# Token product by seven block products instead of eight, with the sums on VectorE

## The reference, cut to what matters

```
x  = attention(q, k, v)                    # 2 x 768 x 512; a band of 96 keys and 8 global keys
t  = x @ w_theta;  zr, zi = x*cos(t), x*sin(t)
y  = w_tok_r @ zr + w_tok_i @ zi           # over the 768 tokens, for each of 2 batches
u  = x + y
v  = u + relu(u @ w_ch)
h  = relu(v @ w_in);  g = h * sigmoid(conv3(h))
out = g @ w_out                            # 2 x 768 x 512
```

## Time and profile before

| | |
|---|---|
| median of 3 runs | 404.9 us (404.44 to 405.19) |
| the profiled execution's own time | 405.32 us |
| its span in the trace | 403.6 us |
| TensorE matmul busy | 396.9 us (98%), 2268 instructions |
| VectorE busy | 214.4 us (53%) |
| ScalarE busy | 215.1 us (53%) |
| GpSimd busy | 130.0 us (32%) |
| DMA moved | 32.17 MB, mean 80 GB/s |

### The profile page before, as it was taken

The page is one execution under the profiler, slowest core; times in us unless marked ns, Lnnn a source line. Parts: engine busy times, 40 slices in busy tenths (PEclk is TensorE's granted clock), DMA queues, the critical chain, the costliest instruction groups (busy, mean ns, idle before and its releaser), DMA issues.

```text
span 403.6 us, 6205 instructions
## 1 busy us (share of the span) xinstructions
PE 396.9 (98%) x2268; PEld 348.2 (86%) x2268; DVE 214.4 (53%) x577; ACT 215.1 (53%) x414; POOL 130.0 (32%) x106
## 2 busy tenths in 40 slices
PE   7999999999999999999999999999999999999996
PEld 2888888898788888888888988999999999999985
DVE  5977777765888643448254421487434435344320
ACT  2777777764787544482333120588555544553531
POOL 2095000001567233265442210248562322222220
PEclk9999999999999999999999999999999999999999
DMA  7964442620000233235420002002100200100022
GB/s 229 417 256 161 162 161 80 144 97 2 0 1 5 101 98 138 78 123 190 132 78 1 2 0 78 28 2 73 31 2 0 80 0 1 52 29 2 0 78 78
DMA packets 12271, 32.17 MB, mean 80 GB/s; under 512 B 4176, under 2 KB 4432, under 8 KB 12240
## 3 DMA queue, kind: packets, MB, share of 16 engines
q1 hardware_dynamic: 12240, 31.77, 22.6%
HBM read 28.62 MB, written 3.15 MB: 79 GB/s over the span
## 4 chain that ended last, share of the span: by engine, by line
PE 96%; ACT 1%; DVE 1%; issue 1%; ACTq 0%
PE bank L453 32%; PE bank L594 24%; PE bank L652 16%; PE bank L500 9%; PE bank L485 6%; PE bank L472 5%; PE bank L565 1%; PE bank L608 1%; PE bank L511 1%; ACT pr L711 1%; DVE trig L1134 0%; ACT trig L779 0%; DVE th_r L1036 0%; DVE bank L1033 0%; DVE xT L1025 0%
## 5 line engine op out<-in xcount | busy, mean ns | idle before, releaser
L594 PE MATMUL bank<-z,wT 128*128 128x512 f32 x432 | 99.3, 390 | 0.0
L594 PEld LDWEIGHTS bank<-z,wT 128*128 128x128 f32 x432 | 80.8, 188 | 16.6
L453 PE MATMUL bank<-vT,win 128*128 128x386 f32 x384 | 73.3, 340 | 0.0
L453 PEld LDWEIGHTS bank<-vT,win 128*128 128x128 f32 x384 | 68.4, 188 | 1.8
L652 PE MATMUL bank<-wout,g 128*128 128x512 f32 x288 | 69.6, 390 | 0.0
L652 PEld LDWEIGHTS bank<-wout,g 128*128 128x128 f32 x288 | 53.9, 188 | 9.7
L1211 DVE SCALAR_TENSOR_TENSOR bank<-h_sb,convw,bank 128x384 f32<-128x384 f32 x32 | 19.9, 622 | 66.7 <-ACT bank L868 66.7
L862 ACT ACTIVATE h_sb<-bank 128x386 f32<-128x386 f32 x32 | 15.8, 493 | 74.0 <-PE bank L453 73.0
L415 POOL TENSOR_TENSOR g<-gf,g 128x384 fp32r<-128x384 f32 x32 | 32.5, 1017 | 68.0 <-ACT g L882 68.0
L500 PE MATMUL bank<-v_sb,pT 128*128 128x65 f32 x352 | 44.6, 268 | 0.0
L500 PEld LDWEIGHTS bank<-v_sb,pT 128*128 128x128 f32 x352 | 43.1, 192 | 0.0
(11 more groups left out here) (77 smaller groups left out, 496.1 us busy)
## 6 DMA issues: line engine op xcount, KB each, us to landing
wrows<-w_tok_laid SPq DMA_DIRECT2D x12, 768.0 KB, 4.4
v_sb<-v_laid SPq DMA_DIRECT2D x8, 780.0 KB, 5.0
qk_sb<-qk_laid SPq DMA_DIRECT2D x7, 792.0 KB, 6.5
out<-ob SPq DMA_DIRECT2D x12, 256.0 KB, 2.2
winraw<-w_in_in SPq DMA_DIRECT2D x4, 512.0 KB, 3.8
woutraw<-w_out_in SPq DMA_DIRECT2D x8, 256.0 KB, 2.7
wthraw<-w_theta_in SPq DMA_DIRECT2D x1, 1024.0 KB, 12.9
wchraw<-w_ch_in SPq DMA_DIRECT2D x1, 1024.0 KB, 5.2
```

Of the source, the lines that this page charges most:

```text
L453: last = pe.matmul(dst, w[a], m[b], start=(i == 0 and j == 0), stop=(i == n - 1 and j == 2))
L594: last = pe.matmul(Y_BANK[s % 2][:], wT[s % 2][:, hi, ri * NT + blk, :], z[b][:, blk, lo, ri, :], start=(blk == 0 and ri == 0 and j == 0), ...
```

## The change

The token product of both batches is written as a product of 2 x 2 blocks: on the left, rows are the two halves of the output tokens (0 and 1, 384 each) and columns the real and imaginary weights; on the right, rows are zr and zi and columns the two batches. Strassen's seven block products take the place of eight. A step `mix_tokens(s)` now has s = 3k + i with k from 0 to 6 (the product) and i from 0 to 2 (the tile in the half); its contraction is 6 blocks long: 18 matmuls of 128 x 512.

- **Left operands.** GpSimd's `prepare(i)` makes, for each i, the seven left operands (five sums or differences and two plain parts) from four raw rows of 768, during the attention: 9 two-input operations and 4 copies of 128 x 768. Six operands stay in SBUF (`a_ops`); five per i are staged, written to a DRAM tensor `a_kept` (`store_a`), and come back in the token stage (`load_a`); the last nine of them come as one part and are split by `high_a` (ScalarE) and `low_a` (VectorE). In exchange SP's `load_w_tok`, `high_rows`, `low_rows` and GpSimd's `split_rows` are gone. `load_v` has three buffers instead of two.
- **Right operands.** `weigh` writes into four raw arrays; `own_difference`, `other_difference`, `sum_six`, `sum_one`, `sum_seven` on VectorE (15 operations of 128 x 1024, SBUF and SBUF) make the sums; `high_b` (ScalarE) and `low_b` (VectorE) split them in 18 pieces of 128 x 1024. The first batch's `high_z` and `low_z` now take 512 columns; the second batch's are gone.
- **Results.** `add_y` adds or subtracts a bank to two tiles of x for k = 0 to 4 and to one for k = 5 and 6.
- **Mixed channels.** v stays in PSUM: `add_mix` is one operation, `high_v` and `low_v` read the bank, `low_v` moves from GpSimd to VectorE; `mix_channels` waits for `low_v`. `high_u` writes a second, unrounded copy (`u_raw`).
- **Orders.** New hand-written orders on TensorE, ScalarE and VectorE. w_in and w_out are loaded later (w_in after the last `low_b`, w_out after the last `add_mix`).

```diff
+        ADDS = (((1, ALU.add), (3, ALU.subtract)), ((1, ALU.add), (0, ALU.add)), ((2, ALU.add), (0, ALU.subtract)),
+                ((2, ALU.add), (3, ALU.add)), ((0, ALU.add), (3, ALU.add)), ((0, ALU.add),), ((3, ALU.add),))
+        B_RAW = (zi[0], zi[1], zd, zr[0], zi[0], zr[1])
...
+            def first_tokens():
+                pe.wait_ge(x_done, NU)
+                pe.wait_ge(staged, NA)
+                for blk in range(NT):
+                    pe.wait_ge(z_lo, blk + 1)
+                    for i in range(NI):
+                        for j, (hi, lo) in enumerate(((0, 0), (0, 1), (1, 0))):
+                            last = pe.matmul(y_bank(i)[:], a_ops[:, i, hi, blk, :], b_ops[:, b_side(0), blk, lo, :], ...)
...
+                for blk in range(NT):
+                    if k >= 1 and i == 0 and blk % 2 == 0:
+                        pe.wait_ge(b_lo, NI * (k - 1) + blk // 2 + 1)
+                    for j, (hi, lo) in enumerate(((0, 0), (0, 1), (1, 0))):
+                        last = pe.matmul(y_bank(s)[:], a_ops[:, slot, hi, blk, :], b_ops[:, side, blk, lo, :], ...)
...
-                if n >= 2:
-                    pe.wait_ge(v_ready, n - 1)
+                if n >= 2:
+                    pe.wait_ge(v_lo, n - 1)
```

GpSimd and its stores:

```diff
+                step(summed(resident(i), w_r1, w_i1, ALU.add))
+                whole(resident(NI + i), w_i1)
+                summed(kept(0), w_r0, w_i0, ALU.add).then_inc(staged, 1)
+                whole(kept(1), w_r0).then_inc(staged, 1)
+                for part, a, b, op in ((2, w_r0, w_i1, ALU.add), (3, w_i0, w_i1, ALU.subtract), (4, w_r1, w_r0, ALU.subtract)):
+                    pool.tensor_tensor(kept(part)[0].bitcast(F32), a, b, op).then_inc(staged, 1)
...
+                prepare(0)
+                prepare(1)
                 split_w_theta()
-                for s in range(2):
-                    split_rows(s)
+                prepare(2)
...
+                for p, count in zip(range(3, NP), (0, 5, 1, 4, 5)):
+                    load_qk(p)
                     load_v(p)
+                    for m in range(kept, kept + count):
+                        store_a(m)
+                        if m == 4:
+                            load_w_raw(2)
```

VectorE's work and its order (the start of it), and ScalarE's wait ahead of the angles:

```diff
+            def low_b(k, two):
+                dve.wait_ge(b_hi, NI * (k - 1) + two + 1)
+                dve.tensor_tensor(b_ops[:, b_side(k), blks, 1, :], B_RAW[k - 1][:, blks, :],
+                                  b_ops[:, b_side(k), blks, 0, :].bitcast(F32), ALU.subtract).then_inc(b_lo, 1)
...
+                dve.scalar_tensor_tensor(out=r, in0=r, scalar=0.0, in1=u_raw[:, j, :], op0=ALU.max, op1=ALU.add)\
+                   .then_inc(v_ready, 1)
...
+            weigh(6)
+            own_difference(0)
+            own_difference(1)
+            own_difference(2)
+            low_b(1, 0)
+            low_b(1, 1)
+            weigh(7)
+            low_b(1, 2)
...
+                if t == 0:
+                    act.wait_ge(staged, NA)
+                    for m in range(4):
+                        act.wait_ge(stored_a[m], 16 * ((NA + 3 - m) // 4))
```

More of the change, by code:

```diff
@@ L28, with build @@
 PI_BELOW = 3.1415925
-def build(nc, q, k, v, qk_laid, v_laid, counts, w_theta, w_tok, w_ch, w_in, conv_w, w_out, out):
+def build(nc, q, k, v, qk_laid, v_laid, counts, w_theta, w_tok, w_ch, w_in, conv_w, w_out, a_kept, out):
     B, H, S, D = q.shape
@@ L634, in hidden @@
                 cols = slice(0, HC) if half == 0 else slice(S - HC, S)
-                product(H_BANK[n % 2][:, 0:HC], [([win[:, part, blk, f * P:(f + 1) * P] for part in range(2)],
+                product(H_BANK[n % 2][:, 0:HC], [([win[blk][:, part, f * P:(f + 1) * P] for part in range(2)],
                                                   [vT[b][:, part, blk, cols] for part in range(2)])
@@ L1153, in _ @@
                     weigh(TRIG_AT[t])
-            for m in range(NT):
-                if m >= 1:
-                    add_y(m - 1)
-                    low_rows(m + 1)
-                weigh(NT + m)
             def low_u(c, blks=range(CB)):
@@ new lines, in _ @@
+            weigh(6)
[6 more added lines that the diff above has]
+            low_b(1, 2)
+            weigh(8)
+            weigh(9)
+            add_y(0)
+            weigh(10)
+            weigh(11)
+            low_b(2, 0)
+            add_y(1)
+            other_difference(0)
+            low_b(2, 1)
+            low_b(2, 2)
+            add_y(2)
+            add_y(3)
+            add_y(4)
@@ L1187, in _ @@
+            add_y(9)
+            sum_one(0)
+            sum_one(1)
+            low_v(1)
+            sum_one(2)
+            low_b(4, 0)
+            add_y(10)
+            add_y(11)
+            low_a(6)
+            low_b(4, 1)
+            low_b(4, 2)
             add_mix(2)
             add_mix(3)
+            low_a(7)
+            low_v(2)
+            low_v(3)
             low_u(1)
-            add_y(8)
-            low_rows(10)
+            add_y(12)
+            sum_seven(0)
+            low_a(8)
@@ L1192, in _ @@
+            sum_seven(1)
+            sum_seven(2)
             add_mix(4)
             add_mix(5)
-            add_y(9)
-            low_rows(11)
+            low_v(4)
+            add_y(13)
+            low_b(5, 0)
+            low_v(5)
+            low_a(9)
+            low_a(10)
+            low_b(5, 1)
+            low_b(5, 2)
+            add_y(14)
+            low_a(11)
+            low_a(12)
+            low_b(6, 0)
+            add_y(15)
+            add_y(16)
+            low_b(6, 1)
@@ L1196, in _ @@
+            low_b(6, 2)
             add_mix(6)
             add_mix(7)
+            low_v(6)
+            low_a(13)
+            add_y(17)
+            low_a(14)
             low_u(2)
-            add_y(10)
-            add_y(11)
+            low_v(7)
+            add_mix(8)
+            add_y(18)
+            low_v(8)
+            add_mix(9)
+            low_v(9)
+            add_mix(10)
+            add_mix(11)
+            low_v(10)
+            low_v(11)
+            add_y(19)
+            add_y(20)
```

581 lines of the change are left out of this document (357 added, 224 removed).

## The result

The changed kernel takes 395.09 us (median of 4 runs, 394.86 to 395.29), the kernel before in the same session 404.67 (404.44 to 405.19): a ratio of 0.976, 95% interval 0.974 to 0.978. The forecast was 394.9. In a later session (5 runs, and 11 of the kernel before) it was 394.74 to 405.07, 0.975 (0.974 to 0.976). With 0.976 in its place the differences to the changed kernel would be 0.4 us smaller, so they are good to about that.

The account below looks back on a forecast made before the run. TensorE was taken as the bound, time being matmuls times the distance of their starts. Saving 12.2 us, less 2.2 of waits, attention at zero, gave -10.0: from 404.9 to 394.9 us, range 392.5 to 399.8.

Parts of the forecast that it names:

- Bound, matmuls removed: Token product: TensorE sets the time; 378 matmuls instead of 432, 54 fewer at 0.2267 us, save 12.2 us.
- VectorE's list: Token stage: VectorE's operations take 93.6 us against TensorE's 114.5, so the order decides; no TensorE wait up to 244.
- The place named as the tightest: Token stage, transpose_u(1): needed at 188.3, add_y(11) there at 187.7, 0.6 us to spare.
- spare of 0.6 to 2 us: Token stage up to 244: how far ahead of TensorE's need the walk had its inputs ready.
- The overlap that I chose: VectorE's list in the token stage: 0.06 us taken off for each of 84 wide operations, 98.6 down to 93.6 us.
- The four late waits: TensorE behind 244: mix_channels(3,0) waits 0.35, mix_channels(3,2) 0.56, hidden(7) 0.40, hidden(8) 0.85; together 2.2 us.
- the last pair: Waits at hidden(7) and (8), 0.40 and 0.85 us, from the relu, taps, sigmoid, gate loop with a w_out split.
- The attention at zero: Attention: GpSimd's three prepares, 19.8 us each from 19.4, end with w_theta at 85 to 87, hidden; cost zero.
- The 0.6 us wait in the angle stage: TensorE's longest wait behind the start-up; the only possible gain there, as high_z and low_z get shorter.
- VectorE as the pace, early or throughout: Rivals: VectorE paces the token stage, part given back (0.24); or it becomes the bound, slower than before (0.04).
- the rival's two parts: Rival (0.24): two-SBUF operations 1.16 times as long lose 3.1 us, hand-overs of 0.15 us lose 2.5; both: 400.5.
- The fall of the clock: Rival (0.02): many small TensorE waits bring one 13 us stretch to 1.2 GHz, costing 13 us: 408.

Follow-up runs that it names:

- before_378: The kernel before with 378 of its 432 token matmuls, one low-by-high product left out for 9 of 12 tiles: 393.29 us, ratio 0.970.
- eighth_product: The changed kernel with the first block product (54 matmuls) computed twice into the same banks: 407.62 us, ratio 1.005 to the kernel before.
- woven_early: The changed kernel with channel mixes between hiddens, early first w_out pieces and splits, and the last two high_u ahead of the first sigmoid: 392.51 us, ratio 0.969.
- woven: The changed kernel with one mix_channels(3,j) between each two of hidden(3) to hidden(8), w_out loaded as late as in the changed kernel: 396.79 us, ratio 0.979.
- prepare_load: The changed kernel with three more two-input operations of 128 x 768 on GpSimd in prepare(2): 400.68 us, ratio 0.988 to the kernel before.
- vector_load: The changed kernel with 12 more VectorE subtractions of 128 x 768, two ahead of each low_b of products 3 and 4: 403.27 us, ratio 0.994.

## Why the prediction was right

- **Bound, matmuls removed.** Right: 54 x 0.2267 = 12.2; before_378 gives 12.1 and eighth_product 12.3.
- **VectorE's list.** Right in sum, and in place but for one: 93.6 foretold, 92.3 us busy between 134 and 244; no wait on TensorE from the first token matmul to `hidden(0)`, which starts at 244.0. The place named as the tightest has the spare foretold: `add_y(11)` ends at 187.1, `transpose_u(1)` starts at 187.75. But there is a tighter one, which the list leaves out and my "spare of 0.6 to 2 us" doesn't cover, and that it went without a wait is partly luck: `mix_channels(2,2)` starts at about 235.7 and needs the `low_v` that ends at 235.5, `mix_channels(2,3)` at about 237.8 one that ends at 237.6. These four mixes follow one another, so v's way through ScalarE and VectorE takes all but 0.2 us of the time; it is the chain that costs 0.4 at `mix_channels(3,2)`. The overlap that I chose, 0.06 a piece, is 0.085 for the `low_b`.
- **The four late waits.** Right: 2.2 foretold, 2.1 by the timeline, 2.2 by woven_early. Of the cause given for the last pair, the late start behind the load holds: with load and splits moved ahead both waits go. That the loop also carries a split doesn't matter: without one its relus are just as far apart, 2.97 us against 2.95.
- **The attention at zero.** Right in the result, and nearly wrong in the reason. A prepare takes 20.6 us (42.50 - 21.88) and not 19.8, from the hand-overs between its operations, and GpSimd starts at 21.9, for it waits for its raw rows behind the other loads, where I had let it start at 19.4. The last operation ends at 90.3 where the sum had 85 to 87, and the sign of being right, done before 90, failed. The last store was to be down at 90; it is down at about 93, and the stage needed it at 93.5. The spare that I gave as 4 us was under a half, and that the cost still came out as nothing is luck: two terms missing from the sum, 2.5 us of hand-overs and a start 2.5 us later, had just used it up. The 0.6 us wait in the angle stage, which I had allowed to go, stayed.
- **Sum and rivals.** 10.0 foretold, 9.6 and 10.3 measured in two sessions. VectorE as the pace, early or throughout, did not come about: its wide operations kept to 1.22 us but for the hits by GpSimd. The upper end of the range, 399.8, also lay below the 400.5 that the rival's two parts give together, though it was to take the rival in. The fall of the clock did not come about in the changed kernel, whose waits are all under a us; it is real, though, as woven and prepare_load show, and I had given it as something that many small waits bring, where here it followed single ones of 2.9 and 4.8 us.

## What to carry to other kernels

Where one engine is at its limit, removed instructions are worth their distance in full, and the work put in their place is free only where the other engine has time left, which the mean over the stage doesn't tell: VectorE had 4% left in one half and 28% in the other, and 11.4 us more of work, two thirds of it in the first, cost 8. (No run loaded the second half, so its room isn't shown.) Walk the ordered lists against each other with durations from rows; here it gave the four waits to 0.2 us. Walk every wait in the source, also those between rows of one kind: the tightest was one that had been left out. An order change should be walked together with the loads that hang on it (woven against woven_early). Where work is taken as hidden under other work, start it from when its data has landed, and add the hand-overs between its own operations.

## What the runs showed that I had not expected

- A wait of TensorE can cost more than itself. After 2.9 us without matmuls (woven) the next 9 took 3.8 us instead of 2.2; after 4.8 us (prepare_load) the next 12 took 4.3 instead of 3.0, with the granted clock at 0.61 and 0.57 of full in those stretches, so at the 1.2 GHz level for part of them. In the changed kernel and vector_load, with waits of 0.4 to 1.4 us, it stayed at full. The Trainium skill, TensorE: Matmul & The Clock Gate, section "HAM oscillation", has the fall to half rate behind waits between bursts of matmuls; the traces agree, here behind one single wait.
- It doesn't come in every run. With the 4.8 us wait the mean clock was below 1 in four runs of four, with the 2.9 us wait in three of six, and there the runs with the fall took 1.7 to 3.1 us more than those without. One kernel then has two times, and its median says little. What decides between the two is not shown.
